# One-hot matrices with two blocks side by side, and the plan of tiles behind the first of them

## What is computed

```python
y = irfft(rfft(x * v) * rfft(h_filt))      # long convolution per channel
x = x * y                                  # attention_out, tokens x 128
# moe: each token goes to one of 8 experts
logits = x @ w_gate + modality_bias[modality_id]
e_idx = argmax(logits)
out[e_idx == e] = gate * (relu(x @ w1[e]) @ w2[e])
# moe2: the same with logits from the normalised token and expert embeddings
```

## Time and profile before

| | us |
|---|---|
| median of 3 runs | 2113.36 (2112.57 to 2116.03) |
| the profiled execution, its own time | 2112.35 |
| its span in the profile | 2110.6 |

### The profile page before, as it was taken

How to read it: one execution, slowest core, us unless ns; L and a number is a source line. 1 busy time by engine, 2 the same in 40 slices (tenths; PEclk the granted TensorE clock), 3 DMA queues, 4 the chain that set the end, 5 groups by cost and what they waited for, 6 DMA issues and landing times. The chain is left out here.

```text
span 2110.6 us, 36683 instructions
## 1 busy us (share of the span) xinstructions
PE 1908.6 (90%) x10191; PEld 1464.8 (69%) x10192; DVE 1418.0 (67%) x3242; ACT 1018.4 (48%) x2043; POOL 908.1 (43%) x879
## 2 busy tenths in 40 slices
PE   8999999999656959999999999984799998999996
PEld 5777677677456637777777777763587786888875
DVE  4759999999726737666766676675555555555554
ACT  1885555555323325555555555553454444454443
POOL 1455455555100026666666666664233332333322
PEclk9999999999878979999999999997899999999998
DMA  2003555555486011111111111124212222111211
GB/s 83 1 25 96 119 120 129 121 120 124 69 202 127 1 53 37 44 42 41 43 44 42 41 41 45 39 61 61 70 45 60 58 64 70 39 49 43 63 38 31
DMA packets 233192, 137.22 MB, mean 65 GB/s; under 512 B 142250, under 2 KB 221044, under 8 KB 232996
## 3 DMA queue, kind: packets, MB, share of 16 engines
q1 hardware_dynamic: 207202, 94.40, 19.4%
q0 software_dynamic: 22080, 39.76, 6.8%
q10 hardware_dynamic: 3842, 2.21, 0.5%
HBM read 95.33 MB, written 43.36 MB: 66 GB/s over the span
## 5 line engine op out<-in xcount | busy, mean ns | idle before, releaser
L1606 DVE SCALAR_TENSOR_TENSOR moe_h_lo<-moe_ph,moe_h_hi 128x512 fp32r<-128x512 f32 x760 | 509.1, 687 | 318.3 <-ACT moe_h_hi L1506 312.6
L1506 ACT ACTIVATE moe_h_hi<-moe_ph 128x512 fp32r<-128x512 f32 x760 | 445.0, 597 | 332.1 <-PE moe_ph L1414 324.5
L1722 POOL DMA_INDIRECT out<-moe_o,moe_idx x200 | 196.0, 980 | 439.0 <-DVE moe_o L1625 374.7
L1410 PE MATMUL moe_po<-moe_h_hi,moe_w_hi 128*128 128x512 f32 x760 | 316.0, 416 | 45.6 <-DVE moe_h_lo L1606 45.4
L1410 PE MATMUL moe_ph<-moe_x_hi,moe_w_hi 128*128 128x512 f32 x760 | 314.8, 414 | 13.3 <-issue 11.3
L1414 PE MATMUL moe_ph<-moe_x_lo,moe_w_hi 128*128 128x512 f32 x760 | 301.2, 396 | 0.0
L1411 PE MATMUL moe_ph<-moe_x_hi,moe_w_lo 128*128 128x512 f32 x760 | 300.8, 396 | 0.0
L1414 PE MATMUL moe_po<-moe_h_lo,moe_w_hi 128*128 128x512 f32 x760 | 300.6, 396 | 0.0
L1411 PE MATMUL moe_po<-moe_h_hi,moe_w_lo 128*128 128x512 f32 x760 | 298.8, 393 | 0.0
L1732 POOL DMA_INDIRECT moe_x<-attention,moe_at x196 | 201.1, 1026 | 226.1 <-issue 215.7
L1722 POOL DMA_INDIRECT rows<-moe_out,moe_r_idx x196 | 195.5, 998 | 189.3 <-ACT moe_out L1521 133.7
(11 more groups left out here) (209 smaller groups left out, 2992.8 us busy)
## 6 DMA issues: line engine op xcount, KB each, us to landing
moe_x<-rows SPq DMA_DIRECT2D x49, 260.0 KB, 2.8
X<-in_x SPq DMA_DIRECT2D x64, 192.5 KB, 5.3
V<-in_v SPq DMA_DIRECT2D x64, 192.5 KB, 4.3
XF<-in_xf SPq DMA_DIRECT2D x64, 192.5 KB, 2.5
r_x<-attention SPq DMA_DIRECT2D x23, 512.0 KB, 6.4
moe_w_raw<-in_moe_w SPq DMA_DIRECT2D x22, 512.0 KB, 3.7
attention<-POOLED SPq DMA_DIRECT2D x48, 220.0 KB
out<-moe_o,moe_idx POOLq DMA_INDIRECT x200, 2.2
```

The lines of the kernel that those rows point to most:

```text
L1410: nc.tensor.matmul(o, hi, m_hi, start=start, stop=False)
L1506: nc.scalar.activation(h_hi[c][:], ph[c % 4][:], ACT.Relu).then_inc(hhi_done, 1)
L1606: nc.vector.scalar_tensor_tensor(out=h_lo[c][:], in0=ph[c % 4][:], scalar=0.0, in1=h_hi[c][:].bitcast(F32), op0=ALU.max, op1=ALU.subtract) ...
L1722: pool.indirect_dma_start(dst, bass.IndirectOffsetOnAxis(ap=idx[:, a:a + 1].bitcast(U32), axis=0), out[:, a, 0:width], None, bounds_check= ...
```

## The change

It does three things. LANES is 2 instead of 4, so that two blocks lie side by side in each one-hot tile and in `count` (416 columns instead of 832); the number of elements that each instruction of the loop handles stays the same. `plan_tiles` is called inside the loop, before the fourth group of one-hots, instead of ahead of the loop. And the last of the GROUPS, of 40 blocks, is cut into one of 32 and one of 8 blocks; by `due` both come in unit 24.

```diff
-LANES = 4
+LANES = 2
...
-    GROUPS = [(0, 48), (48, 48), (96, 48), (144, 40)]
+    GROUPS = [(0, 48), (48, 48), (96, 48), (144, 32), (176, 8)]
...
             ch.settle()
-            plan_tiles(nc, ch, k, counted, planned)
-
             def lanes(x, m, n):
...
             for m in range(NM):
                 q = m % RING
+                if m == RING:
+                    plan_tiles(nc, ch, k, counted, planned)
                 if m >= RING:
                     dve.wait_ge(matched, m - RING + 1)
                     dve.wait_ge(lo_row_done, m - RING + 1)
```

## The result

The changed kernel takes 2094.64 us (median of 4 runs, 2091.97 to 2098.87), the kernel before 2114.7 us (median of 4, 2112.57 to 2116.32). The ratio is 0.9908, with a 95% interval of 0.9888 to 0.9927: about 20 us faster, where 2095.8 us had been forecast. The forecast had been worked out from a median of 2113.36 us, before a fourth run of the kernel before was in. The span of the profiled execution fell from 2110.6 to 2093.1 us, by 17.5.

The account below looks back on a forecast made before the run. PE was taken to bound the one-hot loop, then DVE: start 683.3, groups 49.2, plan 4.0, then PE's tail less 0.3 put the copy at 738.3, 17.6 us earlier, giving a median of 2095.8 us, range 2090 to 2104.

Parts of the forecast that it names:

- The feed of the matmul: One-hot loop on PE: the operands' 8-byte step holds matmuls at 0.188 us; with LANES = 2 they take 0.107 us.
- the row: Profile rows of the one-hot loop: matmuls 0.188 us apart, where the two-hit rule would give 0.087 us.
- DVE as the next bound: One-hot loop: DVE's durations stay, so it bounds at 2.14 us a group, 49.2 us for 23 groups; chance 0.80.
- The second rival: One-hot loop: DVE loses its rate with rows of two elements, 4.07 us a group, 2140 us in all; chance 0.09.
- the fear drawn from section 5.2: One-hot loop: DVE's small operand lacks runs of two adjacent 4-byte words, so it may lose full rate, 26.8 us slower.
- The plan: Plan moved into the loop: with DVE as the bound it costs the same 4.0 us wherever it stands, gain 0.
- The ring: One-hot loop: three groups of buffering cover PE's clock lag and its idle time of about 3.5 us, cost 0.
- The short last group: Last group cut into 32 and 8 blocks: chain takes 10.3 us against 7.25, a loss of 3.0 us.
- The tables and the end: Smaller count table gains 0.3 us; at the loop's end, last lo_first to the copy takes 2.7 us.
- The first rival: One-hot loop: PE stays at 0.188 us because weights' gaps or the clock hold it, 2113.5 to 2114 us; chance 0.07.

Follow-up runs that it names:

- E5: Kernel before with at_hi (moving operand) at two blocks side by side, weights still four, old plan and groups: 2086.95 us beside 2108.95.
- E6: Kernel before with the weights' tiles at two blocks side by side, at_hi still four, old plan and groups: 2107.87 us beside 2108.95.
- E7: Kernel before with LANES = 8 instead of 4, a step of 16 bytes: 2176.11 us beside 2108.95.
- E9: Kernel before with at_hi at a step of 32 bytes (eight blocks in rows of sixteen), weights with two blocks side by side: 2182.56 us beside 2111.29.
- E1: Kernel before with only LANES = 2, plan ahead of the loop and last group of 40 blocks kept: 2090.58 us beside 2110.07.
- E8: Kernel before with LANES = 1, one-hot matrices without gaps: 2132.82 us beside 2108.95.
- E4: Kernel before with LANES = 2 and the plan inside the loop, last group of 40 blocks kept: 2090.34 us.
- E2: Kernel before with only the plan moved inside the loop behind the third group, LANES = 4, old groups: 2107.18 us beside 2110.07.
- E11: Kernel before with LANES = 2 and the plan behind the last one-hot group, last group of 40 blocks kept: 2091.42 us beside 2111.29, ratio 0.9905.
- E3: Kernel before with only the last group cut into 32 and 8 blocks: 2113.62 us beside 2110.07.
- E10: Kernel before with weights at eight blocks side by side (16 bytes) and at_hi at two: 2090.21 us beside 2111.29.

## Why the prediction was right

**The feed of the matmul.** That the spacing of 0.188 us had to be the operand's step, because it did not move with the clock, was right, and E5 and E6 put it on the moving operand. The new spacing of 0.107 us, taken from the 4-byte stream, was too high: it is 0.093 us. It had been worked out that this does not matter below 0.134 us, and it did not. The rule of the page "SBUF — State Buffer", section "The DMA port swizzle" in the Trainium skill (two hits on a 16-byte line are enough) had been weighed against the row. The spacings agree with its 16-byte line and not with its two hits: four hits take 0.093 us (the changed kernel), two take 0.188 (E6), one takes 0.374 (E7, E9).

**DVE as the next bound.** 2.14 us for a group was forecast and found: in E1 no `at_lo` waits for PE, and from the first to the last of them are 22 periods, 682.75 to 729.8 us, 2.14 each. The second rival had its mechanism right and its place one step off: E8 shows the price, 4.07 us a group and 25 us more than before in the loop, but with rows of one element. With rows of two, section 5.1 of "Vector Engine (DVE) Microarchitecture Reference" in the Trainium skill agrees with this case (0.68 us for 1024 elements) and the fear drawn from section 5.2 does not apply to a word that is read again.

**The plan.** Nothing for the move when DVE is the bound (E1 against E4, 0.03 us), 2.6 us when PE is (E2): both as worked out. That it costs the same 4.0 us wherever it stands was too wide: behind the last group DVE waits 1.75 us for PE before the copy, and there E11 hides 1.8 of them. From PE's last start of the third group at 690.35 us to the first of the fourth at 695.05 it was 4.7 us, with about 4.5 of idle time where 3.5 had been expected, and it restarted at a clock of 0.50; the matmuls were 0.17 us apart until the clock rose again, and no `at_lo` waited. The ring covered it.

**The short last group.** 3.0 us were forecast as a loss, 2.7 measured (E3). The slope of 13.0 ns per element was a little low: (7.25 - 3.59)/256 is 14.3, 3.59 us being the chain of the 8 blocks from 673.29 to 676.88, since the narrow instructions beside the wide ones became shorter too. So this term came out 0.3 too high.

**The tables and the end.** 0.3 us had been put down for the smaller `count`. No run shows this term: the stretch from SP's first load to the last group differs by 2.7 us among the profiles, and not by LANES. From the last `lo_first` to the copy 2.42 us, forecast 2.7, for the spacing.

Together: the copy was forecast at 738.3 us and came at 737.39, with 0.47 of the difference from a stage that began earlier. From the first `at_lo` to the copy 55.3 us were forecast (738.6 - 683.3) and 55.04 measured, and that is where the prediction is borne out. What was not in the sum is the stretch behind the copy, 1.0 us longer in this profile and different by up to 6 us among profiles; it made up for the 0.9 us by which the copy came early, and that was luck. The first rival (PE stays at 0.188 us) and the second (DVE falls) did not come about.

## What to carry to other kernels

When a matmul's spacing is the same at both granted clocks, the array isn't what limits it: look at how the moving operand lies, and count how many of its elements share 16 bytes. Choose the interleaving that serves both sides, here the smallest that still leaves DVE two adjacent 2-byte elements. Moving work to a later place in an engine's queue gains only where that engine waits for another one there, as DVE did for PE inside the old loop and still does behind the new one (E11); an edit that was worth 2.6 us before the bound moved was worth nothing after, and a third edit in the same change cost 2.7 us without being seen in the total.

## What the runs showed of the hardware

- The spacings of these matmuls fit a price of about 1.80 ns for each 16-byte line that the moving operand touches, or the array's own time if that is longer. For 208 bf16 columns at a clock of 1.00: no gaps 0.089 us, a step of 4 bytes 0.093, of 8 bytes 0.188. At a clock of 0.50: a step of 4 bytes 0.17, of 8 bytes still 0.19, of 16 bytes 0.374, of 32 bytes 0.374; the last two were never seen at 1.00.
- The weights' step is nearly free beside a moving operand with a step of 4 bytes: recorded loads of 101 ns at 4 bytes (E1), 117 at 8 (E5) and 147 at 16 (E10), with the matmuls at 0.093 to 0.097 us. The record of a load does not depend on its own step alone: at 4 bytes it is 118 ns in E6 and 127 in E9.
- A PE that the profile calls fully busy may stay at the lower clock. In E7 and E9, with matmuls 0.374 us apart, it was "busy" for 40.00 of 40 us and the granted clock stayed at 0.50 through the loop of 140 us; with matmuls 0.188 us apart the clock rose to 1.00 in the kernel before.
- A two-source DVE instruction on bf16 keeps its doubled rate with an operand whose innermost row is two elements (0.68 us for 1024) and loses it with one (1.21 us).
